# Transformer block on one core: channel means as two rounded products, and a new place for the first chunk's normalisation

## What is computed

```python
scores = scale * q @ k.T                      # 8 heads of 64
thresh = max(scores) - tau                    # keep scores >= thresh
x  = softmax(masked scores) @ v               # -> (4, 576, 512)

xk = mu_k * x + (1 - mu_k) * x_prev           # x_prev: x shifted by one position
xr = mu_r * x + (1 - mu_r) * x_prev
x  = sigmoid(xr @ w_r) * (max(xk @ w_k, 0)**2 @ w_v)

u  = x + real(fft(fft(x, axis=1), axis=2))
un = (u - mean(u)) / sqrt(var(u) + 1e-6)      # mean and variance over the 512 channels
out = u + max(un @ w_ch1, 0) @ w_ch2          # 512 -> 2048 -> 512
```

## Time and profile before

| | |
|---|---|
| median of 3 runs | 1093.48 us (1092.77 to 1094.65) |
| profiled execution, its time | 1093.62 us |
| its span in the trace | 1091.8 us |
| granted clock of TensorE, mean | 0.997 |
| busy: PE, DVE, ACT, POOL | 97%, 52%, 47%, 37% |

### The profile page before, as it was taken

The page is one execution under the profiler, slowest core; times in us unless marked ns, Lnnn a source line. Parts: engine busy times, 40 slices in busy tenths (PEclk is TensorE's granted clock), DMA queues, the critical chain, the costliest instruction groups (busy, mean ns, idle before and its releaser), DMA issues.

```text
span 1091.8 us, 18457 instructions
## 1 busy us (share of the span) xinstructions
PE 1057.1 (97%) x7088; PEld 1000.6 (92%) x7088; DVE 570.7 (52%) x1096; ACT 511.4 (47%) x1250; POOL 400.6 (37%) x347
## 2 busy tenths in 40 slices
PE   6999999999999999999999889999999999999998
PEld 6899999998999999999999888888888888888998
DVE  7998765466865566864465755443123223223211
ACT  5988875646875746875656632221111111111110
POOL 5897664423663433563413534331111111111000
PEclk9999999999999999999999989999999999999999
DMA  8634202033302032301123108300200200200000
GB/s 240 186 110 168 57 25 57 3 110 90 101 25 58 18 118 67 101 24 35 45 67 109 44 1 301 122 1 1 70 1 1 70 1 1 69 1 1 36 1 34
DMA packets 43800, 70.10 MB, mean 64 GB/s; under 512 B 4288, under 2 KB 25664, under 8 KB 43200
## 3 DMA queue, kind: packets, MB, share of 16 engines
q1 hardware_dynamic: 43408, 68.59, 20.1%
q10 hardware_dynamic: 304, 0.33, 0.1%
HBM read 56.50 MB, written 12.41 MB: 63 GB/s over the span
## 4 chain that ended last, share of the span: by engine, by line
PE 80%; DVE 10%; ACT 4%; issue 3%; POOL 2%; DMA 0%; SPq 0%; DVEq 0%; ACTq 0%; POOLq 0%
PE PB L780 20%; PE PB L782 20%; PE PB L781 20%; PE PB L840 9%; PE PB L807 6%; PE PB L823 5%; DVE probs L1343 4%; DVE neg_s L1332 2%; ACT mix_v L1145 1%; ACT exps L1074 1%; DVE rowinv L1353 1%; DVE mix_v L1362 1%; ACT mix_h L1160 1%; POOL fold_l L703 1%; DVE k_sq L1432 1%
## 5 line engine op out<-in xcount | busy, mean ns | idle before, releaser
L1288 ACT ACTIVATE h_hi<-PB 128x464 fp32r<-128x464 f32 (+1 forms) x80 | 44.4, 555 | 335.5 <-PE PB L782 335.5
L1530 DVE SCALAR_TENSOR_TENSOR h_lo<-PB,h_hi 128x464 fp32r<-128x464 f32 (+1 forms) x80 | 51.0, 637 | 260.7 <-ACT h_hi L1288 260.7
L840 PE MATMUL PB<-v_sb,probsT 128*128 128x64 f32 (+1 forms) x1440 | 177.5, 270 | 0.0
L840 PEld LDWEIGHTS PB<-v_sb,probsT 128*128 128x128 f32 x1440 | 172.1, 192 | 0.0
L1343 DVE SCALAR_TENSOR_TENSOR probs<-neg_s,thresh,exps 128x576 f32<-128x576 f32 x144 | 156.2, 1084 | 0.2 <-issue 0.2
L1332 DVE TENSOR_SCALAR_CACHE_REDUCE neg_s<-PB,taus 128x576 f32<-128x576 f32 x144 | 117.0, 812 | 47.9 <-PE PB L807 43.7
L1083 ACT ACTIVATE probsT<-PB 128x384 f32<-128x384 f32 (+1 forms) x288 | 109.4, 433 | 68.6 <-PE PB L823 66.8
L780 PE MATMUL PB<-un_h,w1h 128*128 128x464 f32 (+1 forms) x320 | 121.6, 380 | 0.0
L782 PE MATMUL PB<-un_h,w1l 128*128 128x464 f32 (+1 forms) x320 | 118.9, 371 | 0.0
L781 PE MATMUL PB<-h_lo,w2h 128*128 128x464 f32 (+1 forms) x320 | 118.9, 371 | 0.0
L780 PE MATMUL PB<-h_hi,w2h 128*128 128x464 f32 (+1 forms) x320 | 118.8, 371 | 0.0
(11 more groups left out here) (174 smaller groups left out, 2341.2 us busy)
## 6 DMA issues: line engine op xcount, KB each, us to landing
q_raw<-qT_dram SPq DMA_DIRECT2D x62, 160.0 KB, 3.2
k_raw<-kT_dram SPq DMA_DIRECT2D x64, 144.0 KB, 3.1
w_raw<-w_dram SPq DMA_DIRECT2D x8, 1024.0 KB, 9.3
cs<-cs_scr SPq DMA_DIRECT2D x8, 870.0 KB, 6.8
u_scr<-x2T SPq DMA_DIRECT2D x4, 1152.0 KB, 4.8
cd<-cd_scr SPq DMA_DIRECT2D x4, 1032.0 KB, 4.9
v_sb<-v_dram SPq DMA_DIRECT2D x16, 256.0 KB, 2.9
u_in<-u_scr SPq DMA_DIRECT2D x4, 928.0 KB, 5.7
```

What stands on the lines that cost most here:

```text
L840: last = nc.tensor.matmul(bank(6 + p)[:, i * DH:i * DH + width], probsT[:, n % 2, kt * P128:(kt + 1) * P128], v_sb[:, kt, pair % 2, p * DH ...
L1530: nc.vector.scalar_tensor_tensor(h_lo[:, ft % 3, 0:w], bank(4 + ft % 3)[:, 0:w], 0.0, h_hi[:, ft % 3, 0:w].bitcast(F32), ALU.max, ALU.subt ...
```

## The change

It does six things.
1. `part` is also stored in two rounded parts, `part_h` and `part_l`, made by POOL with one rounding and one subtraction behind each sum (`add_tiles`), 10 times. `mean` and `variance` multiply these two by `mean512` read as fp32r (`over_channels`): two products in place of one in plain float32.
2. The chain of chunk 0 in the alone stage stands in another order. POOL: `sum_u(0)` behind `mix_l` 11. PE: `mean(0)` behind r of c = 1, `variance(0)` behind the third group of v. DVE: `center(0)` behind all mixings, at the slot of the first v; `split_w2(0)` behind the y stage. ACT: `square(0)` behind all mixings, `root(0)` later, `norm_hi(0)` behind the fifth k. The table `MIX_AT_ALONE` has mixings 10 to 14 mostly one slot earlier.
3. `fold` begins with the sums: `pair_dif` is made behind the first `fold_v` instead of ahead of it (all 8 folds).
4. The banks of the drain begin with 0 and 1, those in which the scores stood, so that the first two x groups of batch 3 wait for `max_ready` (the last row maximum) and not for the last `y_l`.
5. The eight `wv_low` of the set-up on POOL are spread one by one over slots 35 to 37 and 43 to 47, where they stood in pairs in slots 35, 39, 40 and 44.
6. Waits are counted accordingly.

```diff
-MIX_AT_ALONE = [3, 4, 6, 7, 8, 9, 10, 11, 13, 14, 15, 16, 18, 18, 19, 19]
+MIX_AT_ALONE = [3, 4, 6, 7, 8, 9, 10, 11, 13, 14, 14, 15, 17, 18, 18, 19]
...
-    two, four, six = [... ((2, 3), (2, 3, 0, 1), (6, 5, 0, 1, 2, 3))]
+    two, four, six = [... ((2, 3), (0, 1, 2, 3), (6, 5, 0, 1, 2, 3))]
...
-                    if n in (35, 39, 40, 44):
...
+                    if n in (35, 36, 37, 43, 44, 45, 46, 47):
+                        wv_low(n - 35 if n < 38 else n - 40)
...
                         if stage == "k" and c == 0 and alone(d):
-                            yield 14
+                            yield mix_at(d, 11) + 1
                             pool.wait_ge(u_loaded[0], 16)
...
                     nc.gpsimd.tensor_tensor(part[:, 0, 0:w], part[:, 0, 0:w], part[:, 1, 0:w], ALU.add).then_inc(done, 1)
+                    pool.wait_ge(done, c * 4 + 2)
+                    rounded(part_h[:, 0:w], part[:, 0, 0:w]).then_inc(done, 1)
+                    pool.wait_ge(done, c * 4 + 3)
+                    nc.gpsimd.tensor_tensor(part_l[:, 0:w], part[:, 0, 0:w], part_h[:, 0:w].bitcast(F32), ALU.subtract).then_inc(done, 1)
...
+                def over_channels(c):
+                    w = width_of(c)
+                    nc.tensor.matmul(mean_out(c), mean512[:, :].bitcast(F32R), part_h[:, 0:w], start=True, stop=False)
+                    return nc.tensor.matmul(mean_out(c), mean512[:, :].bitcast(F32R), part_l[:, 0:w], start=False, stop=True)
...
+                        if dt == 0 and alone(d):
+
+                            pe.wait_ge(max_ready, TILES)
...
                                 last.then_inc(r_ready, 1)
+                                if alone(d) and c == 1 and i == 3:
+                                    mean(0)
...
-                                if alone(d) and c == 0 and i == 5:
-                                    mean(0)
...
-                                if alone(d) and c == 0 and i == 1:
+                                if alone(d) and c == 0 and i == 2:
                                     variance(0)
...
                     nc.vector.tensor_tensor(pair_sum[:, :], x2T[:, t, :], x2T[:, 3 - t, :], ALU.add).then_inc(pair_ready, 1)
-                    nc.vector.tensor_tensor(pair_dif[:, :], x2T[:, t, :], x2T[:, 3 - t, :], ALU.subtract).then_inc(pair_ready, 1)
                     nc.vector.memset(fold_v[:, t, 1, ends], 0.0)
-                    dve.wait_ge(pair_ready, d * 4 + t * 2 + 2)
+                    dve.wait_ge(pair_ready, d * 4 + t * 2 + 1)
                     nc.vector.tensor_copy(fold_v[:, t, 0, ends], pair_sum[:, ends])
                     nc.vector.tensor_tensor(fold_v[:, t, 0, near], pair_sum[:, near], pair_sum[:, far], ALU.add).then_inc(fold_ready, 1)
+                    nc.vector.tensor_tensor(pair_dif[:, :], x2T[:, t, :], x2T[:, 3 - t, :], ALU.subtract).then_inc(pair_ready, 1)
+                    dve.wait_ge(pair_ready, d * 4 + t * 2 + 2)
                     nc.vector.tensor_tensor(fold_v[:, t, 1, near], pair_dif[:, near], pair_dif[:, far], ALU.subtract).then_inc(fold_ready, 1)
```

More of the change, by code:

```diff
@@ L179, in bank_turns @@
     of, before, had = {}, {}, {}
-    two, four, six = [itertools.cycle(banks) for banks in ((2, 3), (2, 3, 0, 1), (6, 5, 0, 1, 2, 3))]
+    two, four, six = [itertools.cycle(banks) for banks in ((2, 3), (0, 1, 2, 3), (6, 5, 0, 1, 2, 3))]
     for group in order:
@@ L366, in build @@
         assert early.at <= r.at
+        at = r.at
         part = r.put("part", [P128, 2, W], F32)
+        low = Place(at)
+        part_l, part_h = low.put("part_l", [P128, W], F32R), low.put("part_h", [P128, W], F32R)
+        assert low.at == r.at
         un_h, un_l, sqr, row_stats = [], [], [], []
@@ L1181, in dense @@
                                 nc.scalar.activation(gate_t, gate_t, ACT.Copy, scale=0.5, bias=0.5).then_inc(gate_ready, 1)
-                                if alone(d) and c == 1 and dt == 1:
-                                    square(0)
                         if stage == "k":
@@ L1197, in dense @@
                                 nc.scalar.activation(k_sqh[:, ft, :], k_relu[:, i % 2, :], ACT.Square).then_inc(ksqh_ready, 1)
-                                if alone(d) and c == 1 and ft == 2:
+                                if alone(d) and c == 1 and ft == 4:
                                     norm_hi(0, 0)
@@ L1437, in dense @@
                                     nc.vector.tensor_tensor(k_sql[:, ft, :], k_sq[:, ft, :], k_sqh[:, ft, :].bitcast(F32), ALU.subtract).then_inc(ksql_ready, 1)
-                                if alone(d) and c == 0 and ft == KFT - 1:
-                                    center(0, 0)
                         if stage == "v":
@@ L1442, in dense @@
                                 yield slot_of(d, "v", 0, 0)
-                                split_w2(0, True)
-                                split_w2(0, False)
+                                center(0, 0)
                             for i, dt in enumerate(V_ORDER[c]):
@@ L1453, in dense @@
                                 if alone(d) and c == 0:
[L1454 removed]
+                                    if i == 2:
                                         var_eps(0)
@@ L1477, in dense @@
                                                 y_h[st][0:rows, kind * KC:(kind + 1) * KC].bitcast(F32), ALU.subtract).then_inc(yl_ready, 1)
+                    if alone(d):
+                        split_w2(0, True)
+                        split_w2(0, False)
                     copy, dif, add = sums_of(d)
```

20 lines of the change are left out of this document (8 added, 12 removed).

## The result

The changed kernel takes 1088.80 us, median of 9 runs (1087.09 to 1091.42); the kernel before 1093.33 (1092.77 to 1094.65, 9 runs). The ratio is 0.9957, with a 95% interval of 0.9947 to 0.9967: 4.5 us less, where I forecast 13.9 (1079.6, range 1075.5 to 1084.8). Its profiled execution has a span of 1087.0 us.

The account below looks back on a forecast made before the run. PE, busy 97% of the span, was taken to bound the kernel. Alone stage 8.4, later products 2.9, drain 1.0 and folds 1.6 summed to 13.9 us off 1093.62; with the median 0.14 lower, 1079.6 us, range 1075.5 to 1084.8.

Parts of the forecast that it names:

- nothing, plus or minus 1 us: Set-up on POOL: moving the eight `wv_low` off two busy slots into five later ones changes nothing, plus or minus 1 us.
- I take no fall, since 3.2 us is shorter than the 5 us: Alone stage: the clock holds behind the variance's 3.2 us wait; before, about 5 us passed before it fell.
- a rival (0.14): Alone stage: the clock falls again in the 3.2 us gap, 3 us worse, 1082.7 us; chance 0.14.
- The variance waits 3.2 us: Alone stage, chunk 0: PE waits 3.2 us before the variance instead of 6.6.
- mixings 14 and 15 follow by turns: Alone stage: after `mix_lo` 12 at 617.2, these two mixings run alternately and end at 620.0.
- The alone stage, 8.4 us: From the reordered chain: k of c = 1 starts at 633.2, not 641.56, 8.4 us less if the clock holds.
- Folds, 1.6 us: All folds: earlier `fold_v`, `fold_h` and `fold_l` save 1.6 us of PE's waits for the low part, between 0 and 2.0.
- the first `fold_v` comes earlier: Folds: the first `fold_v` comes one `pair_dif`, 0.67 us, earlier, and so do `fold_h` and `fold_l`.
- Later products 2.9 us: Chunks 1 to 4: 8 products, each 0.37 us cheaper as two rounded ones, save 2.9 us; POOL's added instructions are covered.
- Drain 1.0 us: Drain: the first x transposes no longer wait 0.92 us for the last `y_l`; 1.0 us, floor 0, ceiling 1.2.
- `split_w2(0)` and the squares' additions: Alone stage: with `split_w2(0)` moved behind y at no cost, POOL's additions of squares take 1.19 us, not 3.20.

Follow-up runs that it names:

- e3: The kernel before with only the new slots of the eight `wv_low`; 1097.59 us (1.0033).
- e2: The changed kernel with the folds in their old order, `pair_dif` directly behind `pair_sum`; 1088.27 us (0.9951).
- e1: The changed kernel with the eight `wv_low` back in their old four slots; 1085.24 us (0.9920).
- e9: e1 with a plain fp32 product for the mean of chunk 0, its variance still rounded; 1083.81 us (0.9907).
- e14: The changed kernel itself, timed and profiled again; 1088.77 us (0.9963).
- e6: The kernel before with only the new order of the alone stage's chain, means in plain fp32; 1084.54 us (0.9918).
- e8: e1 with plain fp32 products for mean and variance of chunk 0 alone; 1081.41 us (0.9893).
- e10: e8 with the folds in their old order; 1080.47 us (0.9879).
- e4: The kernel before with only the rounded products, the alone stage in its old order; 1094.03 us (1.0003).
- e12: The changed kernel with each `wv_low` subtraction replaced by a rounding with one SBUF operand (other values, for times alone); 1084.99 us (0.9919).

## Why the prediction was wrong

By its own steps, forecast against measured:

- **`wv_low`, "nothing, plus or minus 1 us": wrong, and the largest miss.** It cost 2.7 to 2.8 us in two profiles of the changed kernel and in e3's, 4.3 in e2's (with the low clock at 99.5 in it), and 3.6 to 3.7 us by medians (e1, e3). I had cited the shared interface for the squares and did not apply it to these eight instructions. Each can hold a mask up for as long as it has left to run, and puts other instructions of POOL beside later masks; in the new places PE waited 1.6 and 1.3 us for what followed, where it was 0.5 us and no wait before.
- **"I take no fall, since 3.2 us is shorter than the 5 us": wrong.** The clock fell behind a wait of 4.1 us, and in e9 behind one of 3.2 us. The case stood there as a rival (0.14) and should have been the forecast. The warning of the Trainium skill ("TensorE: Matmul & The Clock Gate", "Why this matters for your kernels"), that an idle gap between bursts puts the clock back to half, held here at 4.1 us in all 33 runs and at 3.2 us in three of four. The length of the low clock varies, 3.3 us in the first profile, some 7 in e1 and e14. This goes with the spread of the changed kernel's runs, 4.3 us, against 0.9 in e6; the spread's cause was not tested by itself.
- **The variance waits 3.2 us: mis-sized, 4.1.** The step that failed is "mixings 14 and 15 follow by turns": three mixings stood behind the sums, not two. DVE in the changed kernel, ahead of them:

```profile
613.85 1.28 DVE L1449 TENSOR_TENSOR k_sql<-k_sq,k_sqh 128x288 fp32r<-128x288 f32 x1
615.05 1.45 DVE L1444 TENSOR_TENSOR k_sq<-k_relu 128x288 f32<-128x288 f32 x1
616.61 1.27 DVE L1449 TENSOR_TENSOR k_sql<-k_sq,k_sqh 128x288 fp32r<-128x288 f32 x1
617.80 0.82 DVE L1374 SCALAR_TENSOR_TENSOR mix_v<-xT,mus,mix_v 128x288 f32<-128x288 f32 x1
...
620.89 0.51 DVE L1374 SCALAR_TENSOR_TENSOR mix_v<-xT,mus,mix_v 128x288 f32<-128x288 f32 x1
...
624.02 0.74 DVE L1374 SCALAR_TENSOR_TENSOR mix_v<-xT,mus,mix_v 128x288 f32<-128x288 f32 x1 [0.94 <-ACT mix_v L1157]
624.68 2.08 DVE L1388 TENSOR_TENSOR cent<-u_in,PB 128x1856 f32<-128x1856 f32 x1
```

The `mix_v` of mixing 12 came at 617.80, behind `k_sq` and `k_sql` that took 1.27 to 1.45 us each beside POOL's sums, where the same instructions take 0.45 us without them; then mixings 13, 14 and 15 went one by one, to 624.02, and `cent` began at 624.68, 621.7 in the old times and not 620.0. Again instructions of both engines lay side by side.
- **The alone stage, 8.4 us: 5.2.** 0.9 us more of waiting, 1.5 us of low clock, and 0.6 us by which PE was late at the end of the third v group already (0.15 of it from the mean's wait of 0.45 instead of 0.3); 0.2 us are left over. The order itself was worth what I said and more: 9.4 us in e6. The two instructions that the rounding adds, in each of two sums, 3.9 us of chain, ate about half of that, and e8, which leaves them out of chunk 0 alone, has 42.31 us for e1's 47.45. I had counted them in POOL's chain, but not asked what the order would bring without them.
- **Folds, 1.6 us: nothing, or half a microsecond lost** (e2 0.5, e10 against e8 0.9). The step that failed is "the first `fold_v` comes earlier": true, but the wait is for the second low part.
- **Later products 2.9 us: right** (2.9 in the changed kernel and in e4), with the price of 0.43 us a pair for 0.42 forecast. **Drain 1.0 us: right** within the measurement (0.8, not clear of noise by the time alone, 1.1 in the trace). **`split_w2(0)` and the squares' additions: right,** 1.18 us each; in e4, where it still stands beside them, the first took 3.21.

The sum with what was measured: 5.2 + 2.9 + 0.8 - 0.5 - 3.7 = 4.7 us, and 4.5 were measured. So close a match is partly luck: with the alone stage of e14, a second profile of the same kernel (47.51 us, 4.2 less than before), the sum is 3.7.

## What to carry to other kernels

Price a move by what it comes to lie beside, not only by its engine's free time: here the same eight POOL instructions cost 3 to 4 us more in places where a mask began beside them, or beside what they put off, and PE waited for that mask. Where such work has to stand there, short instructions cost less than long ones for the same sum. When an edit makes each product cheaper but lengthens the chain ahead of it, keep it for the places that have cover (chunks 1 to 4, +2.9 us) and leave it out where PE stands waiting (chunk 0, -3.8 us). And a wait of PE has to be closed, not halved: at 4.1 us before the variance the clock still fell in every run, at 3.2 us in three of four, and at 1.44 us or less in none. That is no bound to build on, since in e2's profile it fell in the attention behind a wait of 1.59 us, and behind the same wait in the changed kernel's profile it did not.

## What the runs showed of the hardware that I had not expected

- A POOL subtraction of 128x512 with two SBUF operands took 1.27 us at least, a rounding with one 0.61. A mask of 128x576 on DVE (0.81 us alone) that began beside either took 0.81 us and what the POOL instruction had left less 0.2. The other way round, POOL's subtraction into `wvl` took up to 1.78 us in the changed kernel, the rounding in e12 up to 1.14.
- The granted clock didn't fall while PE stood idle for 4.1 us in the changed kernel (1.00 over 626 to 634) but as it resumed, so the whole price lay on PE's work; in e1, with the same wait (626.16 to 630.25), it was already 0.87 over 626 to 630.
- Two profiles of one kernel differ by 1.4 us within the first ten tiles. A difference of this size in a span is no finding before the place of it is known.
